# Local mask laid into the score banks by matmul, and a reordered end of the first attention batch

## The reference

```
q, k, v: (4, 8, 576, 64)          32 pairs of batch and head
attention on means of 4 tokens:   softmax(qd kd^T / 8) vd, each row repeated 4 times
local attention:                  scores = where(|i - j| < 4, q k^T / 8, -1e9); softmax; times v
x = sum of both                   (2304, 512)
h = x @ w_in1;  g = max(0.01 h, h);  x = g @ w_out1      d_ff = 2048
h = x @ w_in2;  g = h - tanh(h);     out = g @ w_out2
```

## Time and profile before

| | us |
|---|---|
| median of 3 runs | 960.08 (958.05 to 961.69) |
| the profiled execution | 959.57 |
| its span | 957.8 |
| PE busy | 941.6 (98%) |
| DVE, ACT, POOL busy | 547.1, 559.7, 403.3 |
| start of the first up-projection matmul | 48.30 |

### The profile page before, as it was taken

One profiled execution on the slowest core, in us unless ns is written; L12 is line 12 of the kernel. 1 busy time (PEld: TensorE's weight loads), 2 busy tenths in 40 slices (PEclk: granted clock), 3 DMA queues, 4 the chain that ended last, 5 costly groups with the idle time before them and its releaser, 6 DMA issues.

```text
span 957.8 us, 19892 instructions
## 1 busy us (share of the span) xinstructions
PE 941.6 (98%) x7000; PEld 884.0 (92%) x7000; DVE 547.1 (57%) x1098; ACT 559.7 (58%) x1355; POOL 403.3 (42%) x343
## 2 busy tenths in 40 slices
PE   7999999999999999999999999999999999999998
PEld 6799999999999999999999998899899898898997
DVE  6755455535634544553235576776676766766764
ACT  4765546456446455364456677676666666656754
POOL 3584616327236246162442756433233332333232
PEclk9999999999999999999999999999999999999999
DMA  7875111211220121102003113000000000000000
GB/s 156 189 199 140 27 37 41 51 26 25 50 50 24 26 50 26 32 22 67 1 1 102 43 56 88 11 25 1 34 0 0 33 0 0 33 0 0 34 1 33
DMA packets 87797, 41.48 MB, mean 43 GB/s; under 512 B 60352, under 2 KB 81344, under 8 KB 87744
## 3 DMA queue, kind: packets, MB, share of 16 engines
q1 hardware_dynamic: 87744, 40.78, 16.2%
HBM read 36.04 MB, written 4.72 MB: 43 GB/s over the span
## 4 chain that ended last, share of the span: by engine, by line
PE 86%; POOL 4%; ACT 3%; issue 3%; DVE 2%; DMA 0%; SPq 0%; POOLq 0%; ACTq 0%; DVEq 0%
PE ph L531 13%; PE ph L532 13%; PE ph L533 13%; PE acc L607 7%; PE acc L608 7%; PE acc L609 7%; PE acc L560 6%; PE acc L561 6%; PE acc L562 6%; PE banks L429 2%; PE banks L461 2%; PE banks L448 2%; POOL in_lo L1127 1%; PE banks L422 1%; POOL pl L1111 1%
## 5 line engine op out<-in xcount | busy, mean ns | idle before, releaser
L1148 POOL TENSOR_TENSOR g_lo<-scratch,g_hi 128x384 fp32r<-128x384 f32 x96 | 125.8, 1311 | 257.8 <-ACT g_hi L734 257.8
L994 DVE TENSOR_TENSOR ph<-g,ph 128x288 f32<-128x288 f32 x128 | 58.9, 461 | 162.4 <-ACT g L748 161.8
L531 PE MATMUL ph<-x_hi,w_hi_a 128*128 128x288 f32 (+1 forms) x448 | 143.4, 320 | 0.8 <-DVE xT L884 0.5
L533 PE MATMUL ph<-x_hi,w_lo_a 128*128 128x288 f32 (+1 forms) x448 | 140.0, 312 | 0.0
L532 PE MATMUL ph<-x_lo,w_hi_a 128*128 128x288 f32 (+1 forms) x448 | 139.9, 312 | 0.0
L1127 POOL TENSOR_TENSOR in_lo<-w_whole,in_hi 128x512 fp32r<-128x512 f32 x64 | 82.5, 1289 | 131.0 <-ACT in_hi L714 131.0
L748 ACT ACTIVATE g<-ph 128x288 f32<-128x288 f32 x128 | 52.5, 410 | 130.9 <-PE ph L533 130.9
L1132 POOL TENSOR_TENSOR out_lo<-w_whole,out_hi 128x512 fp32r<-128x512 f32 x64 | 86.2, 1347 | 73.8 <-ACT out_hi L718 73.7
L1028 DVE SCALAR_TENSOR_TENSOR scratch<-scratch,ph 128x384 f32<-128x384 f32 x96 | 53.2, 554 | 110.7 <-ACT scratch L797 106.2
L796 ACT ACTIVATE scratch<-ph 128x384 f32<-128x384 f32 x96 | 46.8, 487 | 108.5 <-PE ph L533 106.9
L981 DVE TENSOR_TENSOR g_lo<-ph,g_hi 128x288 fp32r<-128x288 f32 x128 | 58.6, 458 | 59.1 <-ACT g_hi L734 59.1
(11 more groups left out here) (275 smaller groups left out, 2670.6 us busy)
## 6 DMA issues: line engine op xcount, KB each, us to landing
out_dram<-o_stage SPq DMA_DIRECT2D x18, 256.0 KB, 2.1
w_whole<-in_moe_w_in_dram SPq DMA_DIRECT2D x16, 256.0 KB, 3.8
w_whole<-in_moe_w_out_dram SPq DMA_DIRECT2D x16, 256.0 KB, 4.6
qn<-in_q_dram SPq DMA_DIRECT2D x26, 144.0 KB
kn<-in_k_dram SPq DMA_DIRECT2D x26, 144.0 KB
v4n<-in_v_dram SPq DMA_DIRECT2D x26, 144.0 KB
vw<-in_v_dram SPq DMA_DIRECT2D x26, 122.5 KB
scratch<-in_moe_w_in_dram SPq DMA_DIRECT2D x8, 256.0 KB, 2.8
```

The lines of the kernel that those rows point to most:

```text
L531: pe.matmul(bank, whi, x_hi[:, c, 0:width], start=(c == 0), stop=False)
L533: last = pe.matmul(bank, wlo, x_hi[:, c, 0:width], start=False, stop=(c == CD - 1))
L1148: pool.tensor_tensor(g2_lo[:, f % 3, :], g2[:, f % 2, :], g2_hi[:, f % 3, :].bitcast(F32), ALU.subtract).then_inc(g_lo_done, 1)
```

## The change

In the first batch the mask comes into the score banks by PE: `put_mask` multiplies the identity with the band of mask values (`band`, `ident` now typed fp32r, and read as f32 elsewhere; hidden entries are -2^26), 280 columns for bank 1 and 350 for bank 0, and the scores are accumulated on top of it. DVE no longer adds a mask; it takes the maximum of each half in the bank and subtracts from there into `pl`, so bank 0 is freed by the subtraction of its half and not by the mask's addition.

The orders of the four engines are no longer one: `batch0(behind)` takes a table of steps that are moved behind another pair's step, one table for each engine. The copies of steps 12 and 14 of C and D move from ACT to DVE. Kept weights 0 and 1 are split by ACT in slots 22 and 26 and by POOL in 24 and 27, and are loaded ahead of the `vw` loads of C and D. The parts of x are split in slots 27 and 28. `fill` loses 3 and 2 matmuls at step 14 of C and D and gets 2 at step 3 of C. Up-projection banks of the first layer are swapped (`ph1[:, 1 - f % 2]`), and `hidden1(0, 0)` starts when D's bank 1 is free; the waits for D's bank 0 and for B and C stand behind it.

```diff
-KEPT_SLOTS = (24, 27)
-FILL = {("a", 1): 2, ("a", 3): 2, ("b", 1): 1, ("b", 3): 2, ("c", 14): 3, ("d", 14): 2}
-X_HI_SLOTS = {23: (0, 1), 27: (2,)}
-X_LO_SLOTS = {24: (0, 1), 27: (2,)}
+KEPT_HI_SLOTS = (22, 26)
+KEPT_LO_SLOTS = (24, 27)
+FILL = {("a", 1): 2, ("a", 3): 2, ("b", 1): 1, ("b", 3): 2, ("c", 3): 2}
+X_HI_SLOTS = {27: (0, 1), 28: (2,)}
+X_LO_SLOTS = {27: (0, 1), 28: (2,)}
...
+            def placed(slot, at, s):
+                yield slot, at, s, 0
+                for (moved, step), place in behind.items():
+                    if place == (s, at):
+                        yield from placed(slot, step, moved)
...
             load_vw(B, 0, 2)
+            load_kept(0)
             load_vw(C, 0, 4)
+            load_kept(1)
             load_vw(D4, 0, 6)
-            load_kept(0)
-            load_kept(1)
...
+            def put_mask(s, bank):
+                n0, n1 = (0, NBA) if bank == 0 else (NBA, NB)
+                pe.matmul(s.banks[:, bank, 0:(n1 - n0) * WIN], ident_r[:, :], band_r[:, n0:n1, :],
+                          start=True, stop=False)
...
                 elif step == 4:
+                    pe.wait_ge(s.bank_free[1], uses1(i, 2))
+                    if first_of(i):
+                        pe.wait_ge(band_copied, 2)
+                        put_mask(s, 1)
                     pe.wait_ge(s.bank_free[0], uses0(i, 2))
-                    pe.wait_ge(s.bank_free[1], uses1(i, 2))
-                    scores(s)
+                    if first_of(i):
+                        put_mask(s, 0)
+                    scores(s, first_of(i))
...
-                hidden(ph1[:, f % 2, 0:T1], hi, lo, x1_hi, x1_lo, T1, CD * tile if f == 0 else None)
+                hidden(ph1[:, 1 - f % 2, 0:T1], hi, lo, x1_hi, x1_lo, T1, CD * tile if f == 0 else None)
...
-            for _, step, s, i in batch0():
+            for _, step, s, i in batch0({(A, 11): (C, 4), (B, 11): (D4, 4), (C, 15): (D4, 12), (C, 16): (D4, 14)}):
...
+            pe.wait_ge(D4.bank_free[1], uses1(1, 0))
+            hidden1(0, 0)
+            pe.wait_ge(D4.bank_free[0], uses0(1, 0))
-            for s in (B, C, D4):
+            for s in (B, C):
...
                     if first_of(i):
-                        dve.tensor_tensor(s.pl[:, 0:NBA, :], half, band[:, 0:NBA, :], ALU.add)\
-                            .then_inc(s.bank_free[0], 1)
+                        dve.tensor_reduce(s.mxl[:, 0:NBA], half, AX_X, ALU.max).then_inc(s.max_half, 1)
...
+                elif step == 12 and s in (C, D4):
+                    dve.wait_ge(s.bank_full[0], uses0(i, 5))
+                    dve.tensor_copy(s.pT[:, 4:8, :].rearrange("p n q -> p (n q)"), s.banks[0:WIN, 0, 0:4 * P])\
+                        .then_inc(s.bank_free[0], 1)
...
-            for slot, step, s, i in batch0():
+            for slot, step, s, i in batch0({(C, 12): (D4, 9), (A, 15): (C, 14), (A, 16): (A, 15),
+                                            (B, 15): (D4, 12), (B, 16): (B, 15), (C, 15): (B, 16),
+                                            (C, 16): (D4, 14)}):
```

More of the change, by code:

```diff
@@ L269, in batch0, with kept_at @@
                 for at, s in sorted(places, key=lambda place: (place[0] % STEPS >= 6, -(place[0] % STEPS))):
-                    yield slot, at, s, 0
-        def kept_at(slot):
-            return KEPT_SLOTS.index(slot) if slot in KEPT_SLOTS else None
+                    if (s, at) not in behind:
+                        yield from placed(slot, at, s)
+        def kept_at(slots, slot):
+            return slots.index(slot) if slot in slots else None
         def later(f, tile, last):
@@ L430, in score, with scores @@
                                  s.qT[keys, n * QB:n * QB + queries], s.kT[keys, n * QB:n * QB + WIN],
[L431 to L433 removed]
+                                 start=not masked, stop=not masked or at == (NBA, NB - NBA)[bank] - 1)
+            def scores(s, masked):
                 for n in range(NBA - 1):
[L436 to L438 removed]
+                    score(s, 0, n, masked, P if n == 0 and not masked else QB)
+                    score(s, 1, n, masked)
+                score(s, 0, NBA - 1, masked)
                 for n in range(NBA, NB):
[L440 removed]
+                    last = score(s, 0, n, masked)
                     if n == NB - 1:
                         last.then_inc(s.bank_full[1], 1)
[L443 to L444 removed]
+                    score(s, 1, n - 1, masked)
+                score(s, 1, NB - 1, masked).then_inc(s.bank_full[0], 1)
+            def put_mask(s, bank):
+                n0, n1 = (0, NBA) if bank == 0 else (NBA, NB)
+                pe.matmul(s.banks[:, bank, 0:(n1 - n0) * WIN], ident_r[:, :], band_r[:, n0:n1, :],
+                          start=True, stop=False)
             def turn_l(s, bank, n0, n1):
@@ L682, in attention @@
                         .then_inc(s.bank_free[1], 1)
-                elif step == 12:
+                elif step == 12 and s not in (C, D4):
                     act.wait_ge(s.bank_full[0], uses0(i, 5))
@@ L849, in _ @@
                         split_first_x(c)
-                if slot != done and kept_at(slot) is not None:
-                    split_kept(kept_at(slot))
+                if slot != done and kept_at(KEPT_HI_SLOTS, slot) is not None:
+                    split_kept(kept_at(KEPT_HI_SLOTS, slot))
                 done = slot
@@ L1182, in _ @@
             done = -1
-            for slot, step, s, i in batch0():
-                if slot != done and kept_at(slot) is not None:
-                    split_kept(kept_at(slot))
+            for slot, step, s, i in batch0({(D4, 6): (D4, 10)}):
+                if slot != done and kept_at(KEPT_LO_SLOTS, slot) is not None:
+                    split_kept(kept_at(KEPT_LO_SLOTS, slot))
                 done = slot
```

88 lines of the change are left out of this document (35 added, 53 removed).

## The result

The changed kernel took 963.92 us in the median of 19 runs (961.83 to 966.84), the kernel before 960.48 beside it (19 runs): a ratio of 1.0036, 95% interval 1.0025 to 1.0047. The profiled execution took 964.37 us, its span 962.6 (before 959.57 and 957.8).

The account below looks back on a forecast made before the run. PE, busy 98% of the span, bounds the kernel. Shift -2.5 us with the clock up, +0.6 with a full fall; middle -1.0: 959.57 - 1.0 = 958.6, median 0.5 above, 959.1; range 956.4 to 961.8.

Parts of the forecast that it names:

- The mask on PE: Mask matmuls ahead of the scores: 0.17 us for 350 columns, 0.13 for 280; bank 0's on the path, +0.17 a pair.
- my own mark (above 0.2): Sign set beforehand: a mask matmul above 0.2 us would make the prediction wrong.
- DVE's pair and the bank: First batch: DVE's pair 2.4 us instead of 3.15; bank 0 free later, a 1.7 us hole ahead of B's mean product.
- a line through one instruction out of a bank and one out of SBUF: DVE: 350 bank columns at 0.51 us and 630 SBUF columns at 0.82 were said to leave the same fixed part.
- From C's scores to D's mean product: 11.2 us instead of 10.2, giving back the 1.0 won; D's mean product stays near 33.9.
- The first fall of the clock: Clock falls near 19.4 and returns half way: +1.5 us, net -1.0; 40%.
- The end: D's mean product to A's k turn, 16.2 us before: 1.08 + 1.2 + 0.8 = 3.1 saved, then 0.4 wait for ACT's split.
- The lost fills cost nothing.: The fills removed at C 14 and D 14 stood in waits, so losing them costs nothing.
- The end's copies on DVE wait for one another: Rival: DVE's late copies at the end, with dear masks at most +1.5 us on the forecast, 960.6; 6% together.
- dear masks: Rival: mask as dear as float32, 0.5 us a pair for A, B and C; 960.6, 6% together with late copies.
- the 95% for "same": Chance given that the time lies within 0.5% of before (955.3 to 964.9); faster 3%, slower 2%.

Follow-up runs that it names:

- mask_only: Kernel before plus the mask products and DVE's maxima and subtractions in the banks, with all orders, loads, copies and fills of before: 959.95 us, ratio 0.9989.
- vd_back: Changed kernel with POOL's three sums for D's values put back ahead of its product for D's probabilities; ACT's weight splits stay late: 960.20 us, ratio 1.0004.
- pool_early: Changed kernel with POOL's sums for D's values back in the old order and ACT's splits of weights 0 and 1 in slots 22 and 23: 959.88 us, 1.0002.
- split_waits: Changed kernel with POOL's second weight split made to wait until three x_lo are done: 963.51 us, ratio 1.0022.
- fill_hold: Changed kernel with twelve more fill matmuls behind A's query turn, ahead of the first up-projection: 966.72 us, ratio 1.0067.
- best_a: Changed kernel with POOL's first two weight splits in 128x256 pieces, ten fills ahead of B's mean product, twelve ahead of C's last turn: 963.22 us, ratio 1.0025.
- early_fill: Changed kernel with POOL's old order, ACT's two weight splits in slots 22 and 23, and ten fills ahead of B's mean product: 958.56 us, ratio 0.9972.
- mask_pieces: Kernel before with the mask products and POOL's first two weight splits cut into pieces of 128x256: 960.18 us, ratio 0.9994.

## Why the prediction was wrong

- **The mask on PE.** Forecast 0.17 and 0.13 us a bank. Measured, the two stand 0.81 ahead of A's scores at the slow start, 0.48 ahead of D's, so by my own mark (above 0.2) this was wrong. The scores behind it take 1.38 instead of 1.69 at full clock, which I had not foreseen. 0.48 - 0.31 leaves the 0.17 a pair that I had put in the sum: two errors that cancel, which is luck. `mask_only` is level with before.
- **DVE's pair and the bank.** Right, though one argument was unsound: a line through one instruction out of a bank and one out of SBUF cannot compare their fixed parts. With the slope of two bank rows (0.52 at 350 columns, 0.44 at 280, so about 1.1 ns a column) some 0.1 us is left for the subtraction of 350 out of a bank (0.51) and for that of 630 out of SBUF (0.82) alike, so the conclusion stands. A's pair runs from 11.98 to 14.47, 2.49 (forecast 2.4, 3.15). A's mean product was forecast at 12.35; it comes at 12.32 in `mask_only` and 12.20 in `vd_back`. The hole ahead of B's mean product was forecast at 1.7 and is 1.62, in the same place, with DVE as its releaser.
- **From C's scores to D's mean product.** Forecast 33.9, with the clock up. It is 36.54 in the changed kernel's trace, but 33.53 in `vd_back`, which has the same orders on DVE, ACT and PE. The difference is 1.66 of slow start (A's scores end at 11.94 and 10.28) and 1.36 between the mean products of B and C (8.50 and 7.14), where only the changed kernel's trace has the fall.
- **The first fall of the clock.** Taken as a fall with an earlier return; measured 21.3 to 24.6, 3.3 us, at a cost of the 1.36 above where 1.5 was forecast. Right in this trace; in four of the eleven traces with this hole the fall did not come.
- **The end is the step that failed.** I had D's mean product to A's k turn at 16.2 - 3.1 = 13.1 us, with 0.4 more for ACT's split 13.5; it took 17.2 (36.54 to 53.77). The sentence was that DVE does C's copy "only behind D's reciprocal, and PE waits 1.2 there", covered by D's turns. The wait was 1.89, since the scalar operation ahead of that reciprocal stood behind POOL's product. The term missing from the sum is POOL's: the diff moved D's three sums behind D's products and the splits to other slots, and I gave neither a line, not even one that costs them at nothing. The sum had no wait of x_lo for a split either: its pair took 3.35 instead of 0.82. `vd_back` has 15.6 from 33.53 to 49.17, `pool_early` 14.7 from 34.74 to 49.47; so with the wait ahead of C's last turn at 1.07 the end gained 0.6 to 1.5 of the 3.1, x_lo's wait being in both. An estimate: taking off what the pair lost there too (2.69 and 1.79 against 0.82) leaves 13.8 in both, near the 13.5 of the forecast. So the other terms of the end fit, and what the sum lacked is the two holds by POOL, 0.9 us on the 96x3 operation and 2.5 us on x_lo. The rest of the loss came through the clock: from A's k turn to the next wait for POOL the changed kernel took 17.21, with half clock until 58.5, and `vd_back` 15.94.
- **"The lost fills cost nothing."** Not settled: the two kernels with the copies back on ACT had no long hole and fell at 41, where before, with these fills, did not fall. That the fills would have held the clock was not tried.
- **The rivals.** "The end's copies on DVE wait for one another" came nearest, at 6% (together with dear masks) and 960.6: right place, wrong mechanism, and it lacked a second fall of the clock. That the loss stayed below 0.5% fits the 95% for "same".

Still open: what sends 5 of 12 runs of `pool_early` and some of before's to a clock of 0.985 to 0.989, since their profiles caught none of these; the nearest is the trace of `split_waits` with its three falls. Open too is how much of the loss the clock has by itself. It is not all: the seven runs of the changed kernel at 0.995 and 0.996 took 962.6 to 964.7 us, the 51 of before at 0.996 took 959.1 in the median. And level with before is not yet as good as before: `vd_back` had the higher clock (0.9977 against 0.9949 for before beside it), and at 0.996 its five runs took 961.1.

## What to carry to other kernels

When a change moves work on GpSimd, lay its timeline beside VectorE's and mark each VectorE instruction with two SBUF operands, and each small scalar operation out of SBUF, that would begin inside a GpSimd instruction: it ends with that instruction, however small it is itself. (The reciprocals of 96x3 were not held: in before one took its usual 0.17 at 40.22, inside POOL's product of 40.10 to 41.34.) What it costs depends on who waits behind it: 0.95 cost nothing in `mask_only`, and 1.06 stood ahead of PE's next input in the changed kernel. In the profile the sign is one shape with two durations and "issue" in the chain. A wait of TensorE that is short by itself (here 1.9 us) can cost more through the clock behind it. Fills helped where they ended inside the wait (ten ahead of B's mean product) and cost where they did not (`fill_hold`, `best_a`).

## What the runs showed of the hardware

- A 96x3 scalar operation took 1.06 us instead of 0.17 to 0.20, a 128x288 subtraction 2.99 instead of 0.45. They ended 0.03 and 0.32 us behind the GpSimd instruction; the subtraction kept a distance of 0.31 or 0.32 in six traces.
- Eight GpSimd instructions of 0.69 us without a gap held a subtraction that was called in their midst for 2.8 us (3.58 instead of 0.82 for the pair).
- 36 score matmuls that add to a bank filled by a mask product took 1.38 us, the same without it 1.69. Why was not tried.
- Over the 165 runs of before beside the experiments the mean clock runs from 0.985 to 1.000, and the median time with it from 968.2 us (10 runs at 0.985) over 964.4 (13 at 0.989) and 959.1 (51 at 0.996) to 958.4 (20 at 0.998): most of what looks like scatter here is the clock. Not all: the 19 runs at 1.000 took 960.4. The profiled runs of `early_fill` and `mask_pieces`, which began with slow transposes, were the slowest of their kernels' 12 (959.92 and 961.33), and the clock column shows nothing of that start.
